# Four orders of the 21 products of a step in the experts' stage of a gated-attention and mixture-of-experts kernel

## The chip, the cores and the metric

The kernel runs on one core of a Trainium2 chip. The metric is the device time of one execution in microseconds (us), the median of several runs. Everything below is in fp32: each fp32 operand is split into a high and a low part of type fp32r, and a product of two split operands is three matmuls (high by high, and the two mixed terms).

## The reference

The part that the change touches is the last of three stages, the mixture of four experts. It takes 3072 tokens of 384 numbers from the stage before:

```python
def _moe2_ref(x, domain_probs, w1, w2) -> np.ndarray:
    N, D = x.shape
    E = w1.shape[0]
    p = domain_probs / (domain_probs.sum(-1, keepdims=True) + 1e-09)
    out = np.zeros((N, D), dtype=np.float32)
    for e in range(E):
        h = np.maximum(x @ w1[e], 0.0)
        out += p[:, e:e + 1] * (h @ w2[e])
    return out.astype(np.float32)
```

N is 3072, D is 384, E is 4, and the hidden width is 1024. Ahead of it stand a gated linear attention over 4 x 8 heads of 768 steps and a bilinear layer, `((x @ w1) * (x @ w2)) @ w3 @ w_out`.

## The kernel before

The attention and the bilinear layer run interleaved until some 417 us into the span. Then comes the experts' stage, in which TensorE (PE) alternates two kinds of matmul. This text calls them by the letters that the change uses:

- **U** (an "up" or first product, `up2_product`, the matmul at L1175): weights `we_hi` or `we_lo` (128x128), moving operand `x1_hi` or `x1_lo` (128x512), into bank 0 or 1. A step has 9 of them, three contraction tiles by three terms, in the order (x_hi, we_hi), (x_lo, we_hi), (x_hi, we_lo). U0, U1, U2 are the three terms.
- **D** (a "down" or second product, `down2_product`, the matmul at L1294): weights `h_hi` or `h_lo` (128x128, 128 tokens of the hidden activations), moving operand `we_hi` or `we_lo` (128x384). A step has 12 of them: four groups of 128 tokens (`sub` 0 to 3, each summing into its own bank out of 5, 2, 3, 4) by three terms. Sub 0 goes to bank 5, which the profile calls `score_banks`; the others are called `bank`.

For each expert `e` the tokens are taken in 12 tiles of 512 (`TILE2`), two tiles to a round of 16 steps (`STEPS2`), so a tile has 8 steps, one for each 128 hidden units. `step2(e, m, s, ahead)` issues the 12 D of step `s` and the 9 U of the step two further on (`ahead`), which write bank `s % 2`. PE executes its matmuls in the order in which they are written; this order is a literal loop in `step2`. Four experts with 48 tiles make 192 steps. The last two of expert 3 have nothing ahead and hold 12 D alone.

Around the step:

- When the last U of a step is done (`up_done`), ScalarE (ACT, L601) writes `h_hi` from the bank, then VectorE (DVE, L821) writes `h_lo`. PE waits for `h_lo_ready` at the start of the step that uses them, one full step after the U's end.
- In the last step of a tile (`s % 8 == 7`) each token group's last D increments `down_done`, and DVE adds the bank, scaled by the gate, into `total` (`add`, L1000), four adds in the order of the groups. In the first step of the next tile (`s % 8 == 0`) the first D of each group waits for `added`, its own group's add (L1291 ahead of it), since it overwrites the bank. These are the D of index 0, 3, 6 and 9.
- In the very first step, the first D of groups 1 to 3 also wait for `x1_lo_ready`, since their banks hold the end of the stage before, which DVE reads at L816.
- ScalarE and GpSimd (POOL) split the next expert's weights beside this; SyncE loads `x1` tiles two ahead and one weight set an expert.

Of the kernel before, what the change touches and what calls it, by code (L numbers as in the profile page):

```python
# [31 lines left out]
BATCH, HEADS, SEQ, D = 4, 8, 768, 48  # L32
# [11 lines left out]
KT, FT = DM // P, FF // P  # L44
# [11 lines left out]
SUBS = TILE2 // P  # L56
# [9 lines left out]
FOLD_BANKS = [0, 1, 2, 3, 4, 0, 1, 2]  # L66
SUM_BANKS = [5, 2, 3, 4]
TERMS = 3
assert KT * TERMS == SUBS * TERMS - TERMS
WARM = 6  # L70
CONSTANTS = 7
FLAG_STEP = STEPS1 - 4
# [16 lines left out]
def gated_attention_experts(nc, akq, v, akq_long, v_columns, w3T, w_out, wsets, probs, out):  # L89
# [4 lines left out]
    with ExitStack() as ctx:  # L94
# [924 lines left out]
        def _(pe):  # L1019
# [143 lines left out]
            def up2_waits(e, m, s):  # L1163
                u, f = divmod(s, FT)
                if f == 0:
                    pe.wait_ge(x1_loaded[u], 32 * (e * ROUNDS + m + 1))
                    if u == 0 and isinstance(m, int) and m == 0:
                        pe.wait_ge(piece_lo, PIECES * (e + 2))

            def up2_product(e, s, i):  # L1170

                u, f = divmod(s, FT)
                k, term = divmod(i, TERMS)
                cols = slice(k * FF + f * P, k * FF + (f + 1) * P)
                mm = pe.matmul(bank[s % 2][:, :], (we_hi if term < 2 else we_lo)[e % 2][:, cols], (x1_lo if term == 1 else x1_hi)[u][:, k, :],  # L1175
                               start=(i == 0), stop=(i == KT * TERMS - 1))
                if i == KT * TERMS - 1:
                    mm.then_inc(up_done, 1)
# [36 lines left out]
            for k in range(FT):  # L1215
# [5 lines left out]
                for f in range(FOLD_FIRST):  # L1221
# [5 lines left out]
                    else:  # L1227
                        i = k - SPLIT_FROM
# [55 lines left out]
            def down2_product(e, m, s, i):  # L1284

                u, f = divmod(s, FT)
                sub, term = divmod(i, TERMS)
                if term == 0 and e == 0 and s == 0 and sub >= 1:
                    pe.wait_ge(x1_lo_ready, X1_LOW_AHEAD + KT * (TILES1 * BATCH - 1) + sub)
                if term == 0 and f == 0:  # L1290
                    pe.wait_ge(added, SUBS * (e * TILES2 + 2 * m + u) + sub + 1)  # L1291
                rows = slice(sub * P, (sub + 1) * P)
                cols = slice(KT * FF + f * DM, KT * FF + (f + 1) * DM)
                mm = pe.matmul(bank[SUM_BANKS[sub]][:, 0:DM], (h_hi if term < 2 else h_lo)[:, s % 2, rows], (we_lo if term == 1 else we_hi)[e % 2][:, cols],  # L1294
                               start=(f == 0 and term == 0), stop=(f == FT - 1 and term == TERMS - 1))
                if f == FT - 1 and term == TERMS - 1:
                    mm.then_inc(down_done, 1)

            def step2(e, m, s, ahead):

                pe.wait_ge(h_lo_ready, STEPS2 * (e * ROUNDS + m) + s + 1)
                if ahead:
                    up2_waits(*ahead)
                ups = 0
                for i in range(SUBS * TERMS):
                    down2_product(e, m, s, i)
                    if ahead and i % SUBS >= 1:
                        up2_product(ahead[0], ahead[2], ups)
                        ups += 1

            def round2(e, m, following):

                for s in range(STEPS2):
                    if s + 2 < STEPS2:
                        step2(e, m, s, (e, m, s + 2))
                    else:
                        step2(e, m, s, following and (*following, s + 2 - STEPS2))
# [64 lines left out]
```

## Time and profile before

| | us |
|---|---|
| median of 3 runs | 1219.2 |
| lowest and highest | 1218.31 and 1219.39 |
| span of the profiled execution | 1217.6 |
| PE busy in it | 1212.3 |
| experts' stage in it, from the first D to the end | 419.6 to 1217.6 |
| one step of that stage | 4.16 |

The profiled execution has no measured time of its own beside its span. The median of the runs is 1.6 us above the span: what lies around the first and last instruction. In a timeline, the second column is how long a matmul was in the pipeline; matmuls overlap, so what a matmul costs is the distance from its start to the start of the next one.

### The profile page before, as it was taken

How to read it: one execution, taken by the hardware profiler on the slowest of the kernel's cores; microseconds unless marked ns; L12 is line 12 of the kernel's file. 1: busy time of each engine (PE TensorE's matmuls, PEld its weight loads, DVE VectorE, ACT ScalarE, POOL GpSimd, SP SyncE). 2: the span in 40 equal slices, each digit the busy share in tenths (PEclk: the TensorE clock that was granted, in tenths of full speed). 3: DMA queues.
4: the chain of work that ended last, by engine and by line, in shares of the span. 5: the costliest groups of instructions: out<-in, count | busy, mean ns of one | idle time of the engine just before them, and what ended most of it. 6: DMA issues, size and time to landing. Idle time of an engine off the chain costs nothing.

```text
span 1217.6 us, 18865 instructions
## 1 busy us (share of the span) xinstructions
PE 1212.3 (100%) x7740; PEld 1118.6 (92%) x7740; DVE 461.4 (38%) x886; ACT 281.7 (23%) x526; POOL 168.8 (14%) x148
## 2 busy tenths in 40 slices
PE   9999999999999999999999999999999999999998
PEld 8799999999999999999999999999999999999998
DVE  6997586586651122122222222222122222222222
ACT  3443333333333311111111111111111111111111
POOL 1132222222223520000000000000000000000000
PEclk9999999999999999999999999999999999999999
DMA  9644444544415331100141111123101111222201
GB/s 286 207 121 122 126 132 106 137 128 105 126 47 195 106 145 52 51 17 36 53 156 52 52 52 52 52 73 135 42 15 46 52 52 53 78 78 78 78 9 44
DMA packets 87543, 108.03 MB, mean 89 GB/s; under 512 B 38576, under 2 KB 57904, under 8 KB 86960
## 3 DMA queue, kind: packets, MB, share of 16 engines
q1 hardware_dynamic: 87184, 106.63, 28.0%
q8 instruction: 52, 0.85, 0.3%
q10 hardware_dynamic: 288, 0.39, 0.1%
q14 instruction: 19, 0.16, 0.0%
HBM read 86.29 MB, written 18.35 MB: 86 GB/s over the span
## 4 chain that ended last, share of the span: by engine, by line
PE 99%; DVE 0%; issue 0%; DVEq 0%; ACT 0%
PE bank L1175 33%; PE bank L1294 25%; PE bank L1022 9%; PE bank L1024 9%; PE bank L1023 9%; PE score_banks L1294 8%; PE bank L1063 2%; PE bank L1244 1%; PE score_banks L1084 1%; PE bank L1073 1%; PE score_banks L1047 1%; PE bank L1226 1%; PE bank L1214 0%; DVE total L1000 0%; PE bank L1031 0%
## 5 line engine op out<-in xcount | busy, mean ns | idle before, releaser
L821 DVE SCALAR_TENSOR_TENSOR h_lo<-bank,h_hi 128x512 fp32r<-128x512 f32 x192 | 132.8, 691 | 584.9 <-ACT h_hi L601 584.0
L601 ACT ACTIVATE h_hi<-bank 128x512 fp32r<-128x512 f32 x192 | 114.7, 597 | 661.7 <-PE bank L1175 661.7
L1175 PE MATMUL bank<-x_hi,we_lo 128*128 128x512 f32 x576 | 228.7, 397 | 0.0
L1175 PE MATMUL bank<-x_hi,we_hi 128*128 128x512 f32 x576 | 224.1, 389 | 0.0
L1175 PE MATMUL bank<-x_lo,we_hi 128*128 128x512 f32 x576 | 223.5, 388 | 0.0
L1294 PE MATMUL bank<-we_hi,h_hi 128*128 128x384 f32 x576 | 194.6, 338 | 0.0
L1294 PE MATMUL bank<-we_lo,h_hi 128*128 128x384 f32 x576 | 194.5, 338 | 0.0
L1294 PE MATMUL bank<-we_hi,h_lo 128*128 128x384 f32 x576 | 193.8, 336 | 0.0
L499 POOL TENSOR_TENSOR we_lo<-we_raw,we_hi (+1 forms) x48 | 60.9, 1289 | 527.8 <-ACT we_hi L562 527.8
L1175 PEld LDWEIGHTS bank<-x_hi,we_lo 128*128 128x128 f32 x576 | 108.3, 188 | 22.4
L1175 PEld LDWEIGHTS bank<-x_lo,we_hi 128*128 128x128 f32 x576 | 108.0, 188 | 22.7
L1022 PE MATMUL bank<-x,wb_hi 128*128 128x384 f32 x384 | 128.6, 335 | 0.0
L1024 PE MATMUL bank<-x,wb_lo 128*128 128x384 f32 x384 | 128.3, 334 | 0.0
L1023 PE MATMUL bank<-x,wb_hi 128*128 128x384 f32 x384 | 128.3, 334 | 0.0
L1294 PEld LDWEIGHTS bank<-we_hi,h_hi 128*128 128x128 f32 x576 | 108.3, 188 | 8.5
L1294 PEld LDWEIGHTS bank<-we_hi,h_lo 128*128 128x128 f32 x576 | 108.3, 188 | 8.4
L1175 PEld LDWEIGHTS bank<-x_hi,we_hi 128*128 128x128 f32 x576 | 108.3, 188 | 0.2
L1294 PEld LDWEIGHTS bank<-we_lo,h_hi 128*128 128x128 f32 x576 | 108.1, 188 | 0.0
L510 POOL TENSOR_TENSOR g_lo<-g_sb,g_hi 128x384 fp32r<-128x384 f32 x64 | 66.3, 1036 | 221.3 <-ACT g_hi L591 221.3
L811 DVE TENSOR_TENSOR g_sb<-a_sb,bank 128x384 f32<-128x384 f32 x64 | 35.3, 552 | 110.8 <-PE bank L1024 110.8
L1022 PEld LDWEIGHTS bank<-x,wb_hi 128*128 128x128 f32 x384 | 72.1, 188 | 0.2 <-issue 0.2
L1023 PEld LDWEIGHTS bank<-x,wb_hi 128*128 128x128 f32 x384 | 72.1, 188 | 0.1
(99 smaller groups left out, 1473.3 us busy)
## 6 DMA issues: line engine op xcount, KB each, us to landing
x_hi<-x_hi_spill SPq DMA_DIRECT2D x24, 768.0 KB, 4.8
x_lo<-x_lo_spill SPq DMA_DIRECT2D x24, 768.0 KB, 6.3
we_raw<-wset SPq DMA_DIRECT2D x4, 3072.0 KB, 10.0
inputs<-akq SPq DMA_DIRECT2D x24, 448.0 KB, 5.2
values<-v_rows SPq DMA_DIRECT2D x24, 256.0 KB, 3.7
inputs<-akq SPq DMA_DIRECT2D x24, 224.0 KB, 3.3
x_hi_spill<-x_hi_out SPq DMA_DIRECT2D x8, 576.0 KB, 4.3
x_lo_spill<-x_lo_out SPq DMA_DIRECT2D x8, 576.0 KB, 5.2
```

The lines of the kernel that those rows point to most:

```text
L499: pool.tensor_tensor(set_lo(n)[:, at], set_raw(n)[:, at], set_hi(n)[:, at], ALU.subtract).then_inc(piece_lo, 1)
L510: pool.tensor_tensor(g_lo[:, s % 2, :], g_sb[:, s % 2, :], g_hi[:, s % 2, :], ALU.subtract).then_inc(g_lo_ready, 1)
L601: act.activation(h_hi[:, s % 2, :], bank[s % 2][:, :], ACT.Relu).then_inc(h_hi_ready, 1)
L811: dve.tensor_tensor(g_sb[:, s % 2, :], a_sb[:, s % 2, :], bank[1][:, 0:TILE1], ALU.mult).then_inc(g_ready, 1)
L821: dve.scalar_tensor_tensor(out=h_lo[:, s % 2, :], in0=bank[s % 2][:, :], scalar=0.0, in1=h_hi[:, s % 2, :], op0=ALU.max, op1=ALU.subtract) ...
L1022: pe.matmul(dst, left[0], right[0], start=first, stop=False)
L1023: pe.matmul(dst, left[0], right[1], start=False, stop=False)
L1024: return pe.matmul(dst, left[1], right[0], start=False, stop=last)
L1047: mm = pe.matmul(bank[5 + half][rows, STATE_AT + i * D:STATE_AT + (i + 1) * D], keys_t[:, pair, rows], values[:, c % SLOTS, at], start=(i ...
L1063: mm = pe.matmul(bank[7][q * ODD:(q + 1) * ODD, (2 * row + g) * CHUNK:(2 * row + g + 1) * CHUNK], values[:, c % SLOTS, at], scores[:, row, ...
L1175: mm = pe.matmul(bank[s % 2][:, :], (we_hi if term < 2 else we_lo)[e % 2][:, cols], (x1_lo if term == 1 else x1_hi)[u][:, k, :], start=(i ...
L1294: mm = pe.matmul(bank[SUM_BANKS[sub]][:, 0:DM], (h_hi if term < 2 else h_lo)[:, s % 2, rows], (we_lo if term == 1 else we_hi)[e % 2][:, cols],
```

## The change

The loop over the 12 D of a step, in which a U followed each D whose index is 1, 2 or 3 modulo 4, becomes a loop over a string of letters, one string for each expert:

```diff
-assert KT * TERMS == SUBS * TERMS - TERMS
+ORDERS = [7 * "D" + "DU" + 4 * "DUU", 3 * "DDDUU" + "DDDUUU", 3 * "D" + 3 * "DDU" + 3 * "DUU", 3 * "D" + 3 * "DDDUUU"]
+assert all((weave.count("D"), weave.count("U")) == (SUBS * TERMS, KT * TERMS) for weave in ORDERS)
...
-                ups = 0
-                for i in range(SUBS * TERMS):
-                    down2_product(e, m, s, i)
-                    if ahead and i % SUBS >= 1:
+                ups = downs = 0
+                for product in ORDERS[e]:
+                    if product == "D":
+                        down2_product(e, m, s, downs)
+                        downs += 1
+                    elif ahead:
                         up2_product(ahead[0], ahead[2], ups)
                         ups += 1
```

Written out, the order of a step of 21 products is:

```
before, all experts  DDUDUDU DDUDUDU DDUDUDU
after, expert 0      DDDDDDDD U D UU D UU D UU D UU
after, expert 1      DDD UU DDD UU DDD UU DDD UUU
after, expert 2      DDDDD U DD U DD U D UU D UU D UU
after, expert 3      DDDDDD UUU DDD UUU DDD UUU
```

The kinds, counts, operands and order among the D and among the U are the same; every order ends with a U, as before. Other engines' instructions do not change.

```order
L1294 MATMUL score_banks<-we0_hi,h_hi 128x384
L1294 MATMUL score_banks<-we0_lo,h_hi 128x384
L1175 MATMUL bank0<-x1_0_hi,we0_hi 128x512
L1294 MATMUL score_banks<-we0_hi,h_lo 128x384
L1175 MATMUL bank0<-x1_0_lo,we0_hi 128x512
L1291 REGISTER_ALU
L1294 MATMUL bank2<-we0_hi,h_hi 128x384
L1175 MATMUL bank0<-x1_0_hi,we0_lo 128x512
L1294 MATMUL bank2<-we0_lo,h_hi 128x384
L1294 MATMUL bank2<-we0_hi,h_lo 128x384
```

The same place after; the lines have moved by one:

```order
L1295 MATMUL bank3<-we0_hi,h_hi 128x384
L1295 MATMUL bank3<-we0_lo,h_hi 128x384
L1176 MATMUL bank0<-x1_0_hi,we0_hi 128x512
L1295 MATMUL bank3<-we0_hi,h_lo 128x384
L1176 MATMUL bank0<-x1_0_lo,we0_hi 128x512
L1176 MATMUL bank0<-x1_0_hi,we0_lo 128x512
L1292 REGISTER_ALU
L1295 MATMUL bank4<-we0_hi,h_hi 128x384
L1176 MATMUL bank0<-x1_0_hi,we0_hi 128x512
L1176 MATMUL bank0<-x1_0_lo,we0_hi 128x512
```

Before these stand six D, of groups 0 and 1. So the first U stands behind eight D instead of two, and the first D of group 3 (the wait that is nearest to its release) is the 13th product of the step instead of the 16th.

On PE, the same step in the loop of expert 3, after:

```order
L1295 MATMUL bank2<-we1_hi,h_hi 128x384
L1295 MATMUL bank2<-we1_lo,h_hi 128x384
L1295 MATMUL bank2<-we1_hi,h_lo 128x384
L1176 MATMUL bank0<-x1_0_hi,we1_hi 128x512
L1176 MATMUL bank0<-x1_0_lo,we1_hi 128x512
L1176 MATMUL bank0<-x1_0_hi,we1_lo 128x512
L1292 REGISTER_ALU
L1295 MATMUL bank3<-we1_hi,h_hi 128x384
```

Before, this place reads as the first fence does, with `we1` for `we0`. Three terms of a token group now stand together, and three U of a contraction tile behind them.

## Rows read from the trace of the kernel before

**Rows 1.** The page: busy time by engine, granted PE clock, the chain that ended last.

```profile
PE 1212.3 (100%) x7740; PEld 1118.6 (92%) x7740; DVE 461.4 (38%) x886; ACT 281.7 (23%) x526; POOL 168.8 (14%) x148
PEclk9999999999999999999999999999999999999999
PE 99%; DVE 0%; issue 0%; DVEq 0%; ACT 0%
```

**Rows 2.** The waits: engine and line, who released it: us, times, longest.

```profile
ACT h_hi L601 <- PE bank L1175: 661.7, 192, 3.8
DVE h_lo L821 <- ACT h_hi L601: 584.0, 170, 3.7
...
PEld score_banks L1294 <- DVEq L1010: 0.4, 1, 0.4
```

**Rows 3.** The timeline of PE around one step: start us, us, engine, line, op.

```profile
548.69 0.34 PE L1294 MATMUL score_banks<-we_hi,h_hi 128*128 128x384 f32 x1
...
552.45 0.34 PE L1294 MATMUL bank<-we_hi,h_lo 128*128 128x384 f32 x1
552.62 0.40 PE L1175 MATMUL bank<-x_hi,we_lo 128*128 128x512 f32 x1
552.85 0.34 PE L1294 MATMUL score_banks<-we_hi,h_hi 128*128 128x384 f32 x1
553.03 0.34 PE L1294 MATMUL score_banks<-we_lo,h_hi 128*128 128x384 f32 x1
553.20 0.39 PE L1175 MATMUL bank<-x_hi,we_hi 128*128 128x512 f32 x1
553.43 0.34 PE L1294 MATMUL score_banks<-we_hi,h_lo 128*128 128x384 f32 x1
553.61 0.39 PE L1175 MATMUL bank<-x_lo,we_hi 128*128 128x512 f32 x1
553.84 0.34 PE L1294 MATMUL bank<-we_hi,h_hi 128*128 128x384 f32 x1
554.01 0.40 PE L1175 MATMUL bank<-x_hi,we_lo 128*128 128x512 f32 x1
554.24 0.34 PE L1294 MATMUL bank<-we_lo,h_hi 128*128 128x384 f32 x1
```

**Rows 4.** The same timeline, the first D of the second and of the 191st step.

```profile
423.89 0.34 PE L1294 MATMUL score_banks<-we_hi,h_hi 128*128 128x384 f32 x1
...
1210.13 0.34 PE L1294 MATMUL score_banks<-we_hi,h_hi 128*128 128x384 f32 x1
```

**Rows 5.** The same timeline where nine U, then nine 384-column products stand.

```profile
413.76 0.39 PE L1175 MATMUL bank<-x_hi,we_hi 128*128 128x512 f32 x1
413.98 0.39 PE L1175 MATMUL bank<-x_lo,we_hi 128*128 128x512 f32 x1
414.21 0.40 PE L1175 MATMUL bank<-x_hi,we_lo 128*128 128x512 f32 x1
414.45 0.40 PE L1175 MATMUL bank<-x_hi,we_hi 128*128 128x512 f32 x1
...
415.85 0.34 PE L1022 MATMUL bank<-g_hi,wp_hi 128*128 128x384 f32 x1
...
417.41 0.39 PE L1175 MATMUL bank<-x_hi,we_hi 128*128 128x512 f32 x1
```

**Rows 6.** The timeline with the weight loads (PEld), inside a step.

```profile
700.19 0.39 PE L1175 MATMUL bank<-x_hi,we_hi 128*128 128x512 f32 x1
700.19 0.19 PEld L1294 LDWEIGHTS bank<-we_hi,h_hi 128*128 128x128 f32 x1
700.41 0.34 PE L1294 MATMUL bank<-we_hi,h_hi 128*128 128x384 f32 x1
700.42 0.19 PEld L1175 LDWEIGHTS bank<-x_lo,we_hi 128*128 128x128 f32 x1
```

**Rows 7.** The timeline of the other engines around a tile's end: start us, us.

```profile
550.78 0.62 DVE L1000 SCALAR_TENSOR_TENSOR total<-bank,gate,total 128x384 f32 x1
551.99 0.62 DVE L1000 SCALAR_TENSOR_TENSOR total<-bank,gate,total 128x384 f32 x1 [0.59 <-PE bank L1294]
552.97 0.62 DVE L1000 SCALAR_TENSOR_TENSOR total<-bank,gate,total 128x384 f32 x1 [0.36 <-PE bank L1294]
553.05 0.60 ACT L601 ACTIVATE h_hi<-bank 128x512 fp32r<-128x512 f32 x1 [3.56 <-PE bank L1175]
553.68 0.69 DVE L821 SCALAR_TENSOR_TENSOR h_lo<-bank,h_hi 128x512 fp32r<-128x512 f32 x1
```

**Rows 8.** The timeline at the start of the stage: the last readers of banks 2 to 4.

```profile
418.19 1.49 DVE L816 TENSOR_TENSOR x_lo_out<-bank,x_hi_out 128x384 fp32r<-128x384 f32 x3 [0.82 <-ACT x_hi_out L597]
...
419.62 0.45 PE L1294 MATMUL score_banks<-we_hi,h_hi 128*128 128x384 f32 x1
```

## Prediction of the change's effect, made before its run

> **What bounds the kernel now.** I read the page first. PE is busy for 1212.3 of 1217.6 us, at full granted clock in every slice, and 99% of the chain that ended last is PE's [rows 1]. The waits say the same from the other side. The other engines wait for PE: ScalarE's h_hi waited 661.7 us in total for the first products, 192 times. The only wait of PE's weight loads in the experts' stage is 0.4 us, once, at its start [rows 2]. So a reordering on PE can matter in two ways only: PE may take longer or shorter for the same 21 products, or a wait may appear that is now satisfied in time.
>
> Next the timeline. A step of the experts' stage takes 4.16 us: one step's first D starts at 548.69, the next one's at 552.85 [rows 3]. This holds for the whole stage. The second step starts at 423.89 and the 191st at 1210.13 [rows 4], which is 786.24 us over 189 steps, 4.160 each, with loop ends, tile ends and changes of expert inside. There is no bubble anywhere to win back, so one nanosecond more or less a step, over the 190 changed steps, is 0.19 us.
>
> **What a product costs.** In the step, from start to start, a D costs 0.17 to 0.18 us and a U 0.22 to 0.23 [rows 3]. How do the two kinds cost when each stands alone in a run? The end of the stage before has that [rows 5]. Nine products of 384 columns run from 415.85 to 417.41, 1.56 us, 0.1733 each. They have D's shape and run just behind nine U, so I take them for D. Of the nine U the last six run from 414.45 to 415.85, 1.40 us, 0.2333 each. The first three run from 413.76 to 414.45, 0.69 us, 0.23 each: a U run starts a little cheap. Priced at the run's rates a step is 12 x 0.1733 + 9 x 0.2333 = 2.08 + 2.10 = 4.18 us. The mixed step takes 4.16, so mixing saves 20 ns of 4180. That is all that order has been worth so far.
>
> Why so little? Each weight load starts when the matmul ahead of it starts and no sooner: the load for the D at 700.41 starts at 700.19 together with the U, and the load for the next U at 700.42 with the D [rows 6]. A load takes 0.19 us and only one is ahead. Neither kind can then lend its slack to the other, and the sum is nearly independent of the order.
>
> The Trainium skill, page "TensorE: Matmul & The Clock Gate", section "Back-to-back issue gap", says that the spacing of a stream of load and matmul pairs is set by both, pipelined through a window of 64 entries. Taken at its word, loads could run several products ahead, a mix of U and D would even out, and runs of D would lose. The trace bears this out only for one load ahead, so by the rows the sum below stands, and by the page runs would cost up to what mixing now saves, which is the first rival.
>
> **The change, part by part.** Nothing is removed or added; 12 D and 9 U stand in another order in 190 steps, 48 for each of experts 0 to 2 and 46 for expert 3. The last two steps hold D alone and are the same as before.
>
> (a) *PE's own rate.* The known points of the saving against 4.18 are these. The step before has three groups of DDUDUDU and saves 20 ns, 6.7 for each [rows 3, 4]. The run of nine U and nine D takes 417.41 - 413.76 = 3.65 us against 9 x 0.4067 = 3.66, so it saves up to 10 ns (the rows' last digit is 10 ns) for one group of D followed by one group of U [rows 5]. Both fit this: about 6.7 ns are saved each time that U begins behind at least two D, and none where a lone D stands between two U. That is a fit to two patterns, not a mechanism, but it is the nearest thing that the rows offer. By it:
>
> - expert 0, one such place (eight D, then U): 4.180 - 0.007 = 4.173, +13 ns a step;
> - expert 1, four places (DDD each time): 4.180 - 0.027 = 4.153, -7 ns;
> - expert 2, three places (DDDDD, DD, DD): 4.160, 0;
> - expert 3, three places: 4.160, 0.
>
> The sum is 48 x (13 - 7) ns = +0.3 us. The four pairs behind a lone D in expert 0 and the three in expert 2 are patterns that the trace lacks. Their bounds: they save as much as any other start (6.7 ns each), or nothing. I take nothing, since the lone D of the step before, the nearest rows, fit that.
>
> (b) *The wait for the adds.* In a tile's first step the first D of each token group waits for that group's add. The tightest is group 3. Before, its last D starts at 552.45, its add starts at 552.97 and ends at 553.59, that is 0.74 us into the new step [rows 3, 7]. Its first D of the new tile is the 16th product. After, the group's last D stands ahead of two U in experts 0 and 2 and of three in 1 and 3, 0.6 or 0.9 us before the step's end instead of 0.4, so the add ends at about 0.5 or 0.3 us. The 10th D is wanted after 9 D and 3 U in experts 0 and 2, 9 x 0.173 + 3 x 0.23 = 2.25 us, and at some 2.9 us in the others. Spare time is over 1.7 us. The adds of groups 0 to 2 run inside the old tile's last step. The second starts at 550.78, 2.09 us into that step, and ends at 2.71 [rows 7]; the third can follow at once, since group 2's last D then stands at 2.3 us at the latest in the new orders, and ends at about 3.4 of the 4.16. So group 1 is released some 1.4 us and group 2 some 0.7 us before the new step, and the soonest that they are wanted is 0.52 and 1.04 us into it (expert 0, after three and after six D). The cost is nothing. Behind such a wait the whole rest of PE's queue would stand, and behind that ScalarE and VectorE.
>
> (c) *The wait for h_lo.* Every order ends with a U, as before. h_hi starts at 553.05, h_lo at 553.68 and ends at 554.37 [rows 7]; it is wanted at 552.85 + 4.16 = 557.01. The spare is 2.6 us and doesn't move.
>
> (d) *The very first step.* The first D's of groups 1 to 3 come earlier, but their banks' last readers end at 418.19 + 1.49 = 419.68, and the step's first D starts at 419.62 [rows 8]. Group 1's first D now comes 0.5 us after that. The cost is nothing.
>
> (e) The loads of x1, the weight splits and the adds follow semaphores that come at the end of a step or a tile, as before. Nothing moves that they wait for by more than 0.5 us, and none of them is on PE's path.
>
> **The sum.** 1217.6 + 0.3 = 1217.9 us of span, and with the 1.6 us around it 1219.5. I predict 1219.5, no difference that can be measured. A measurement of this kernel tells about 0.2%, 2.4 us, from no change; that would take 13 ns a step on average over all the changed steps.
>
> **Rivals.**
>
> 1. *Short alternation is what saves the 20 ns; groups pay the run's rates.* Each step then takes 4.18: + 0.020 x 190 = 3.8 us, 1223.0 and slower by 0.3%. For it speaks that the later U of a long run cost 0.233 and none in the mix costs that on average; three of the orders have pairs or triples. Against it, the first three U of the run together are still at 0.69 instead of 0.70 [rows 5], and no group here is longer than three. It decides for slower from an average step of 4.173 on, two thirds of the way. Chance 0.15.
>
> 2. *Every change from D to U saves 6.7 ns in the new patterns, behind a lone D too.* Expert 0 has five such places (4.147), expert 1 four (4.153), expert 2 six (4.140), expert 3 three (4.160): 48 x (-13 - 7 - 20) ns = -1.9 us, 1217.3. Against it: in the step before there are nine such changes and only 20 ns. This is still within 0.2%. Chance 0.15.
>
> 3. *Pairs of U are cheap in a way that neither run nor mix shows.* The first U of a run costs 0.22 [rows 5]; were all nine at 0.227 and all D at 0.1733, a step would be 4.12, -0.040 x 190 = -7.6 us, 1211.6. Against it, the third U of the run costs 0.24. Chance of getting a third of this or more, which is faster by over 0.2%: 0.06.
>
> 4. *A wait for an add takes over.* It needs the release of group 3 later than 2.25 us into a tile's first step; it costs what is beyond that, in 24 tiles. By (b) it is 1.7 us away. Chance 0.01.
>
> 5. *The order does nothing at all* and the step stays at 4.160 everywhere: 1219.2. Chance 0.15.
>
> **How the numbers follow.** The forecast has 0.48. With rivals 2 and 5 the chance of no measurable difference is 0.78, slower is rivals 1 and 4, 0.16, and faster is rival 3, 0.06. The range goes from rival 2, 1217.3, to rival 1, 1223.0; it leaves out rival 3, rival 4 and what noise lies beyond the ends.
>
> **What would show it.** In the profile after, PE's step by expert: the distance between first D's should be 4.17, 4.15, 4.16 and 4.16 us. If all are at 4.18, rival 1 holds. The wait view should still show one wait of PE for 0.4 us in the experts' stage and nothing behind the adds. A U's time in the group UUU should be 0.22, 0.23, 0.24 as at 413.76. The prediction is wrong if any order's step is off by over 20 ns from its figure, or if gaps stand ahead of the D that wait for adds.

## The result and the profile after

The changed kernel takes 1223.17 us, the median of 5 runs (1222.45 to 1223.43), against 1218.74 for the kernel before (1218.29 to 1219.39). The ratio is 1.0031, with a 95% interval of 1.002 to 1.0042. It is slower by 4.4 us. The profiled execution has a span of 1221.5 us, 3.9 more than before. The two figures differ because the profiled execution of the kernel before, with 1217.6 us, was some 0.5 us longer than the median of its runs gives (1218.74 less the 1.7 that lie around the span).

The page after, the lines that answer to [rows 1]:

```profile
PE 1216.2 (100%) x7740; PEld 1119.3 (92%) x7740; DVE 458.3 (38%) x886; ACT 282.0 (23%) x526; POOL 168.9 (14%) x148
PEclk9999999999999999999999999999999999999999
PE 99%; DVE 0%; issue 0%; DVEq 0%; ACT 0%
```

PE still sets the end, at full clock, and is busy for 3.9 us more than in [rows 1], with the same 7740 matmuls. The waits after, which answer to [rows 2]:

```profile
ACT h_hi L602 <- PE bank L1176: 665.2, 192, 3.8
...
PEld score_banks L1295 <- DVEq L1011: 0.4, 1, 0.4
```

The one wait of 0.4 us at the start of the experts' stage is still the only one there. So no wait was added, and the whole loss is in how long PE takes for the same products.

Where? The distances between the first D of successive steps tell it. These are rows of PE's timeline after (start us, us): the first D of the second step, of the first step of experts 1, 2 and 3, and of the 191st step. They answer to [rows 4].

```profile
424.02 0.34 PE L1295 MATMUL score_banks<-we_hi,h_hi 128*128 128x384 f32 x1
...
620.48 0.34 PE L1295 MATMUL score_banks<-we_hi,h_hi 128*128 128x384 f32 x1
...
820.15 0.34 PE L1295 MATMUL score_banks<-we_hi,h_hi 128*128 128x384 f32 x1
...
1020.81 0.34 PE L1295 MATMUL score_banks<-we_hi,h_hi 128*128 128x384 f32 x1
...
1213.99 0.34 PE L1295 MATMUL score_banks<-we_hi,h_hi 128*128 128x384 f32 x1
```

| expert | order | from to | steps | us a step | over before |
|---|---|---|---|---|---|
| 0 | 8D U D UU D UU D UU D UU | 424.02 to 620.48 | 47 | 4.180 | +20 ns |
| 1 | DDDUU three times, DDDUUU | 620.48 to 820.15 | 48 | 4.160 | 0 |
| 2 | 5D U DD U DD U D UU D UU D UU | 820.15 to 1020.81 | 48 | 4.180 | +20 ns |
| 3 | 6D UUU, DDD UUU twice | 1020.81 to 1213.99 | 46 | 4.200 | +40 ns |

Experts 0 to 3 lose 47 x 20, 0, 48 x 20 and 46 x 40 ns: 0.94 + 0.96 + 1.84 = 3.7 us. The second step's start is 0.13 us later than in [rows 4], which makes nearly all of the 3.9.

The order of expert 3 costs more than the rates of both runs together (4.18). A step of it, from the timeline:

```profile
1104.79 0.34 PE L1295 MATMUL score_banks<-we_hi,h_hi 128*128 128x384 f32 x1
1104.96 0.34 PE L1295 MATMUL score_banks<-we_lo,h_hi 128*128 128x384 f32 x1
1105.14 0.34 PE L1295 MATMUL score_banks<-we_hi,h_lo 128*128 128x384 f32 x1
1105.32 0.35 PE L1295 MATMUL bank<-we_hi,h_hi 128*128 128x384 f32 x1
1105.50 0.34 PE L1295 MATMUL bank<-we_lo,h_hi 128*128 128x384 f32 x1
1105.68 0.34 PE L1295 MATMUL bank<-we_hi,h_lo 128*128 128x384 f32 x1
1105.86 0.39 PE L1176 MATMUL bank<-x_hi,we_hi 128*128 128x512 f32 x1
...
1106.55 0.34 PE L1295 MATMUL bank<-we_hi,h_hi 128*128 128x384 f32 x1
...
1107.77 0.34 PE L1295 MATMUL bank<-we_hi,h_hi 128*128 128x384 f32 x1
...
1108.99 0.34 PE L1295 MATMUL score_banks<-we_hi,h_hi 128*128 128x384 f32 x1
```

The two groups DDDUUU last 1107.77 - 1106.55 = 1.22 us each, exactly the run rates (3 x 0.1733 + 3 x 0.2333). The six D from 1104.79 to 1105.86 take 1.07 us instead of 1.04. The fourth, fifth and sixth cost 0.18 us each, though nothing stands between them and they are D like the others.

The wait for the adds went as foreseen. These are the last add of a tile in expert 0, then two of PE's rows: the first D of the new tile's first step, and the D that waits. They answer to [rows 7].

```profile
520.05 0.62 DVE L1001 SCALAR_TENSOR_TENSOR total<-bank,gate,total 128x384 f32 x1 [0.97 <-PE bank L1295]
```

```profile
520.16 0.34 PE L1295 MATMUL score_banks<-we_hi,h_hi 128*128 128x384 f32 x1
...
522.42 0.34 PE L1295 MATMUL bank<-we_hi,h_hi 128*128 128x384 f32 x1
```

The last add ends at 520.67, 0.51 us into the step, and the 10th D starts at 522.42, 2.26 us into it.

### The profile page after: what moved, and what is told of

It reads as the page before. It is cut to its first block, busy times and chain, and to the rows that moved or that the text cites. A ratio compares the mean times of both kernels' runs of the same rounds, so it can differ in the third digit from the quotient of the medians.

```text
span 1221.5 us, 18865 instructions
## 1 busy us (share of the span) xinstructions
PE 1216.2 (100%) x7740; PEld 1119.3 (92%) x7740; DVE 458.3 (38%) x886; ACT 282.0 (23%) x526; POOL 168.9 (14%) x148
## 4 chain that ended last, share of the span: by engine, by line
PE 99%; DVE 0%; issue 0%; DVEq 0%; ACT 0%
PE bank L1176 33%; PE bank L1295 25%; PE bank L1023 9%; PE bank L1025 9%; PE bank L1024 9%; PE score_banks L1295 8%; PE bank L1064 2%; PE bank L1245 1%; PE score_banks L1085 1%; PE bank L1074 1%; PE score_banks L1048 1%; PE bank L1227 1%; PE bank L1215 0%; DVE total L1001 0%; PE bank L1032 0%
## 5 line engine op out<-in xcount | busy, mean ns | idle before, releaser
L1176 PE MATMUL bank<-x_lo,we_hi 128*128 128x512 f32 x576 | 226.4, 393 | 0.0
```

## The experiments

In each experiment but two, a kernel gives every expert an order of its own, so that one run prices four orders. A step's price is the distance between the first D of neighbouring steps inside an expert, averaged over the expert, since the rows shown have only 10 ns. It repeats to 1 ns from step to step, unless said otherwise. The exception is an expert's first step, which runs behind another order and can be up to 25 ns off. All runs had the full clock. The kernels of four orders were run once each; the two kernels of one order at the end, several times.

### Is it the order, or the expert?

The theory after the result was that the order alone sets the step. The rival was that the expert does (its weight buffer, or the loads and splits beside it).

```diff
-ORDERS = [7 * "D" + "DU" + 4 * "DUU", 3 * "DDDUU" + "DDDUUU", 3 * "D" + 3 * "DDU" + 3 * "DUU", 3 * "D" + 3 * "DDDUUU"]
+ORDERS = ["DDDDDDUUUDDDUUUDDDUUU", "DDDDDDDDUDUUDUUDUUDUU", "DDDUUDDDUUDDDUUDDDUUU", "DDDDDUDDUDDUDUUDUUDUU"]
```

> The four orders of the changed kernel given to other experts: expert 0 takes expert 3's, expert 1 takes 0's, expert 2 takes 1's, expert 3 takes 2's. Theory A, the order alone sets the step: 4.20, 4.18, 4.16, 4.18 us for experts 0 to 3, span about 1221.5. Theory B, the expert does (its weight buffer, or what the other engines do beside it): 4.18, 4.16, 4.18, 4.20 as in the changed kernel.

Measured: 4.200, 4.180, 4.160 and 4.180 us, span 1220.7. The steps add up as in the changed kernel (790.04 us from the second to the 191st, against 789.97); the span is 0.7 us shorter because the second step starts at 423.25 instead of 424.02. The price goes with the order. Two neighbouring steps of expert 0, which now has the order of expert 3:

```profile
507.25 0.34 PE L1295 MATMUL score_banks<-we_hi,h_hi 128*128 128x384 f32 x1
...
511.45 0.34 PE L1295 MATMUL score_banks<-we_hi,h_hi 128*128 128x384 f32 x1
```

This excludes the weight buffers and the work beside an expert.

### Is it the place in the step?

```diff
+ORDERS = ["DDDUUUDDDDDDUUUDDDUUU", "DDDUUUDDDUUUDDDDDDUUU", "DDDUUUDDDUUDDDUUDDDUU", "DDDDUUUDDDDUUUDDDDUUU"]
```

> Expert 0: DDDUUU DDDDDDUUU DDDUUU; expert 1: DDDUUU DDDUUU DDDDDDUUU (both are the changed kernel's expert 3 shifted against the step's start). Theory A, the cyclic order alone counts: 4.20 us both. Theory B, the place of the six D against the step's start (semaphore waits, h_hi and h_lo of the other engines) counts: 4.18 us or less, since the stall then has no cause. Expert 2: DDDUUU DDDUU DDDUU DDDUU, expert 1's order shifted: 4.16 by A. Expert 3: DDDDUUU three times: if the excess of 20 ns comes of the long D run behind UUU, between 4.18 and 4.24; if only of six D in a row, 4.18.

Measured: 4.200 and 4.200, 4.160, and in expert 3 steps of 4.213 and 4.187 us in turn, 4.200 on average. The shift changes neither price. The stall moves with the six D, to other banks, other operands, and another time against h_hi, h_lo and the adds. That excludes the semaphores and the other engines' work, and that one bank is slower than another. The change of bank still falls behind the third of the six D in both shifts; the next run moves that too.

Expert 3 is the most telling. Its input is one block, DDDDUUU, over and over, and the blocks come out unequal:

```profile
1114.85 0.34 PE L1295 MATMUL score_banks<-we_hi,h_hi 128*128 128x384 f32 x1
...
1115.55 0.39 PE L1176 MATMUL bank<-x_hi,we_hi 128*128 128x512 f32 x1
...
1116.24 0.34 PE L1295 MATMUL bank<-we_lo,h_hi 128*128 128x384 f32 x1
...
1116.95 0.40 PE L1176 MATMUL bank<-x_hi,we_hi 128*128 128x512 f32 x1
...
1117.65 0.34 PE L1295 MATMUL bank<-we_hi,h_lo 128*128 128x384 f32 x1
```

The first block lasts 1.39 us (four D in 0.70, three U in 0.69), the second 1.41 (0.71 and 0.70). They go on in turn, and since a step has three blocks, its length alternates too. At the run rates both would be 1.393. So the price of a block depends on what came before it. PE carries something over from block to block.

The changed kernel shows the same without any repetition, where the order changes. These are the first, second and third step of expert 3, the first behind the last step of expert 2:

```profile
1020.81 0.34 PE L1295 MATMUL score_banks<-we_hi,h_hi 128*128 128x384 f32 x1
...
1024.99 0.34 PE L1295 MATMUL score_banks<-we_hi,h_hi 128*128 128x384 f32 x1
...
1029.19 0.34 PE L1295 MATMUL score_banks<-we_hi,h_hi 128*128 128x384 f32 x1
```

The same 21 products in the same order take 4.18 us behind expert 2's order (4.177) and 4.20 behind their own. Expert 1's first step takes 4.155 (then 4.160) and expert 2's 4.197 (then 4.180); the same pairs of orders in the rotated kernel give 4.155 and 4.196. It isn't the change of expert itself: in the kernel below whose four experts all have expert 3's order, each expert's first step takes 4.200 like the rest.

### Do prices of blocks add?

The prediction had added up block prices. Five runs tried that.

```diff
+ORDERS = ["DDUDDUDDUDUDUDUDUDUDU", "DDDDUDUDUDUDUDUDUDUDU", "DUDUDUDUDDDDUDUDUDUDU", "DDUUDDUUDDUUDDUUDDDDU"]
```

> Four new patterns. Expert 0: DDU three times, then DU six times; expert 1: DDDD, then DU eight times, then U behind the last D; expert 2: DU four times, DDDD U, DU four times; expert 3: DDUU four times, DDDDU. By the prediction's fit (6.7 ns saved for each U group behind two or more D): 4.160, 4.173, 4.173, 4.147 us. By whole steps of 20 ns, as the changed kernel's rows show them: only 4.14, 4.16, 4.18 or 4.20 can come out.

Measured: 4.167, 4.200, 4.200 and 4.167 us. All four miss the fit's figures, by 7 to 27 ns. They miss the steps of 20 ns too: 4.167 is 6.7 ns above 4.160. Experts 1 and 2 have the same cyclic order and the same price. In them DU by itself costs 0.407, which is the sum of the run rates; plain alternation saves nothing. In both, the first three D of DDDD cost 0.174, 0.175 and 0.177 us and the fourth 0.185, though the bank changes ahead of the fourth D in expert 1 and ahead of the third in expert 2. So the change of bank isn't the cause either.

```diff
+ORDERS = ["DDDDDDDDDDDDUUUUUUUUU", "DDDDDDUUUUDDDDDDUUUUU", "DDDUDDDUUDDDUUUDDDUUU", "DDUUDDUUDDUUDDUDDDDUU"]
```

> Expert 0: twelve D, then nine U. Expert 1: DDDDDD UUUU DDDDDD UUUUU. Expert 2: DDD U DDD UU DDD UUU DDD UUU. Expert 3: DDUU DDUU DDUU DDU DDDDUU. If run rates alone price a run, expert 0 is 4.18 us (less 0.007); if a D run behind a U run of three or more pays 20 ns each time, expert 0 is 4.20, expert 1 is 4.22, expert 2 is 4.18, expert 3 is 4.16.

Measured: 4.173, 4.193, 4.173 and 4.193 us. The first is the figure of the run rates; the theory of 20 ns for each D run behind three or more U misses all four, by 7 to 33 ns. Twelve D and nine U cost what the run rates say less 7 ns, as the nine and nine in [rows 5] do. The stall is not a matter of long runs: none of the twelve D behind nine U is slow. In expert 1 the six D behind four U pay it, and the six behind five U don't.

Three further runs looked for shorter steps:

```diff
+ORDERS = ["DDUDUUDDDUUDDDUUDDDUU", "DDDUUDDUDDDUUDDUDDUUU", "DDUUDDDUUDDUDDDUUDDUU", "DDUUDDUUDDUUDDDUUDDDU"]
```

> Four further orders. The rows of the changed kernel and of the first experiments give block prices against run rates: DDDUU saves 7 ns, DDUDUDU saves 7, DDU saves up to 7, a closing UUU none. By those: DDUDUU DDDUU DDDUU DDDUU 4.153 us (if its first block saves as the others), DDDUU DDU DDDUU DDU DDUUU 4.153 to 4.160, DDUU DDDUU DDU DDDUU DDUU 4.153 to 4.160, DDUU DDUU DDUU DDDUU DDDU 4.160 to 4.167. If prices of blocks don't add, values from 4.15 to 4.20 come in no such order.

Measured: 4.153, 4.173, 4.160 and 4.167 us. Three are in their range; the second misses by 13 ns.

```diff
+ORDERS = ["DDUDUDUDDDUUDDDUUDDUU", "DDUDUDDUDUDDUDUDDUDUU", "DDUDDUDDDUUDDDUUDDUUU", "DDDDUUDDDUUDDUUDDUUDU"]
```

> Four more. DDUDUDU DDDUU DDDUU DDUU: 4.153 to 4.160 us by block prices. DDUDU three times, DDUDUDDUDUU in all twelve D and nine U: 4.153 to 4.167. DDUDDU DDDUU DDDUU DDUUU: 4.153 to 4.160. DDDDUU DDDUU DDUU DDUU DU: 4.160 to 4.173. If prices of blocks don't add: anything from 4.15 to 4.20.

Measured: 4.167, 4.153, 4.160 and 4.187 us. Two are in their range. The last is off by 13 ns and the first by 7.

```diff
+ORDERS = ["DDUDUUDDUDUDDDUUDDDUU", "DDUDUDDDUUDDUDUUDDDUU", "DDUDUDDUDUDDUDUUDDDUU", "DDDUUDDDUUDDDUUDDUUDU"]
```

> Four orders made of DDUDU, DDUDUU and DDDUU. If each of these blocks saves 7 ns against run rates, as the two orders of 4.153 us suggest, all four orders are at 4.147 to 4.153 us, the last (DDDUU three times, DDUU DU) at 4.153 to 4.160. If prices of blocks don't add, some are at 4.16 or above.

Measured: 4.160, 4.153, 4.153 and 4.160 us. The first two have the same four blocks in another sequence and differ by 7 ns. So prices of blocks don't add. That the misses are small here may come of the choice of blocks, which had been cheap together; this wasn't tried.

The 29 orders of these and the main kernels (a few are shifts of one another) lie between 4.153 and 4.200 us, 1.1% apart, and every one, once it repeats, is a multiple of 6.67 ns (4.153, 4.160, 4.167 and so on). So are the run rates of D and U, 26 and 35 times. The first step of an expert need not be (4.155, 4.197). The time of 16 columns at the granted 2.4 GHz is 6.67 ns; that the two belong together is a guess.

### What sets the price of a D?

The prediction had explained the small effect by the weight loads: one load ahead, 0.19 us long, about as long as a D. If a D lasts as long as its load, fewer columns in a D would save nothing. Experts 0 to 3 have the order of before and the changed kernel's of experts 0, 1 and 3.

```diff
+ORDERS = ["DDUDUDUDDUDUDUDDUDUDU", "DDDDDDDDUDUUDUUDUUDUU", "DDDUUDDDUUDDDUUDDDUUU", "DDDDDDUUUDDDUUUDDDUUU"]
...
+                width = DM if f == 0 else 320
+                cols = slice(cols.start, cols.start + width)
-                mm = pe.matmul(bank[SUM_BANKS[sub]][:, 0:DM], (h_hi if term < 2 else h_lo)[:, s % 2, rows], (we_lo if term == 1 else we_hi)[e % 2][:, cols],
+                mm = pe.matmul(bank[SUM_BANKS[sub]][:, 0:width], (h_hi if term < 2 else h_lo)[:, s % 2, rows], (we_lo if term == 1 else we_hi)[e % 2][:, cols],
```

> Experts 0 to 3 run the order of before, then the changed kernel's orders of experts 0, 1 and 3. Each D moves 320 columns instead of 384, except in a tile's first step; the last 64 output columns lack those products. Theory L, a D lasts as long as its weight load and its columns hide behind that: D stays at 0.173 to 0.175 us and the four steps at 4.16, 4.18, 4.16 and 4.20. Theory M, a D is paid by its columns: by the slope between 384 and 512 columns (0.1733 to 0.2333) it falls by 0.03 us, and a step by 12 x 0.03 = 0.36, to 3.80 to 3.84. If the differences of 20 ns between the orders come of D's and U's reads meeting, they change or vanish; if of the loads alone, they stay.

Measured, in steps with the narrow D: 3.820, 3.853, 3.820 and 3.847 us (the last 3.829 and 3.864 in turn). Behind a tile's first, wide step the next two differ in expert 0, 3.831 and 3.815, so what is carried over can outlast a whole step. The eight D of expert 1's order, the first, the second and the U behind the last of them:

```profile
684.32 0.31 PE L1297 MATMUL score_banks<-we_hi,h_hi 128*128 128x320 f32 x1
684.47 0.31 PE L1297 MATMUL score_banks<-we_lo,h_hi 128*128 128x320 f32 x1
...
685.49 0.40 PE L1176 MATMUL bank<-x_hi,we_hi 128*128 128x512 f32 x1
```

The weight loads of the second term of groups 1 to 3, in the same run (shortest, median and longest in ns):

```profile
L1297 PEld LDWEIGHTS bank<-we_lo,h_hi x576: 187/188/192, 422.0 to 1160.7; 128*128 128x128 f32 x192
```

Eight D in 1.17 us are 0.146 each, 0.027 less than at 384 columns, exactly what 64 columns take at 2.4 GHz. Theory L falls: the load does not hold a D back, although each load is still recorded with 0.188 us. The kernel before already spoke against it: there a D costs 0.173 and its load is recorded with 0.19. Theory M is right on the kind of bound, but it took the slope from D to U for the price of a column, 0.030 for 64; it is 0.027, and the rest of the distance from D to U is something that a U of 512 columns pays besides. So experts 1 and 3 lie above its 3.84. The differences between the four orders went from 0, 20, 0 and 40 ns to 0, 33, 0 and 27, so the loads alone, which are the same, don't make them.

### Does it hang on the length of a U?

```diff
-                mm = pe.matmul(bank[s % 2][:, :], (we_hi if term < 2 else we_lo)[e % 2][:, cols], (x1_lo if term == 1 else x1_hi)[u][:, k, :],
+                width = TILE2 if term == 0 else 448
+                mm = pe.matmul(bank[s % 2][:, 0:width], (we_hi if term < 2 else we_lo)[e % 2][:, cols], (x1_lo if term == 1 else x1_hi)[u][:, k, 0:width],
```

> The same four orders. The second and third term of each U moves 448 columns instead of 512; the last 64 tokens of each tile lack those terms. Both theories: such a U costs 0.20 instead of 0.23 us, since that is above a load, and the step falls by 6 x 0.027 to 6 x 0.030 = 0.16 to 0.18 us. Theory L leaves the differences between the four orders as they are (0, 20, 0, 40 ns); if they hang on U's length, they change.

Measured: 4.007, 3.993, 3.993 and 4.000 us, in the same four orders. The step falls by 0.153, 0.187, 0.167 and 0.200 us, where 0.16 to 0.18 was expected of every order. The ranking turns over: the order of before is now the slowest of the four, and the differences to it are 0, -13, -13 and -7 ns. No order is good or bad in itself, then. The ranking holds for the widths with which it was measured.

Another run made eight of the nine U as wide as a D; the matmul's line is changed as above:

```diff
+                width = TILE2 if i == 0 else DM
```

> The four orders of before and of the changed kernel's experts 0, 1 and 3, with eight of the nine U at 384 columns, as wide as a D; only a step's first U has 512. The last 128 tokens of each tile lack the products left out. If the differences between the orders come of U being longer than D, they shrink with it: 20 x 0.1733 + 0.227 to 0.233 us = 3.693 to 3.700 in all four orders, at most 7 ns apart. If they come of something that each product has whatever its width (its weight load, its bank, its place), they stay at 0, 20, 0 and 40 ns.

Measured: 3.713, 3.733, 3.720 and 3.713 us. Steps of experts 1 and 3:

```profile
675.91 0.33 PE L1296 MATMUL score_banks<-we_hi,h_hi 128*128 128x384 f32 x1
...
679.65 0.33 PE L1296 MATMUL score_banks<-we_hi,h_hi 128*128 128x384 f32 x1
```

```profile
1033.25 0.34 PE L1296 MATMUL score_banks<-we_hi,h_hi 128*128 128x384 f32 x1
...
1036.97 0.34 PE L1296 MATMUL score_banks<-we_hi,h_hi 128*128 128x384 f32 x1
```

Neither expectation holds. The spread shrinks from 40 to 20 ns but is not gone, and all four are 13 ns or more above the 3.700 that was expected at most. The order of expert 3, the worst at full width, is here the best together with that of before. That the one long U among twenty equal products does it isn't shown, since no run had all 21 equal. This run was inconclusive on the mechanism.

### The whole kernel on one order

```diff
+ORDERS = ["DDDDDDUUUDDDUUUDDDUUU", "DDDDDDUUUDDDUUUDDDUUU", "DDDDDDUUUDDDUUUDDDUUU", "DDDDDDUUUDDDUUUDDDUUU"]
```

> All four experts run DDDDDD UUU DDD UUU DDD UUU, the changed kernel's expert 3. If the order's price is the whole cause, and holds for every expert: a step of 4.200 us, 40 ns over before, 190 steps, + 7.6 us, a ratio of 1.0062. If the changed kernel's loss came of the changes between experts or of something else, it would stay near 1.003.

Measured: 1226.86 us against 1219.12, a ratio of 1.0062 with an interval of 1.0049 to 1.0076. The expected ratio was 1.0062. Its step is 4.200 in all four experts: from the second to the 191st step,

```profile
424.18 0.34 PE L1295 MATMUL score_banks<-we_hi,h_hi 128*128 128x384 f32 x1
...
1217.98 0.34 PE L1295 MATMUL score_banks<-we_hi,h_hi 128*128 128x384 f32 x1
```

793.80 us over 189 steps. The price of the order, 7.6 us over 190 steps, is the whole of the loss of 7.7, within the interval.

```diff
+ORDERS = ["DDUDUUDDDUUDDDUUDDDUU", "DDUDUUDDDUUDDDUUDDDUU", "DDUDUUDDDUUDDDUUDDDUU", "DDUDUUDDDUUDDDUUDDDUU"]
```

> All four experts run DDUDUU DDDUU DDDUU DDDUU, the shortest step found so far, 4.153 us. By the order's price: - 6.7 ns in 190 steps, - 1.3 us against before, a ratio of 0.9990, which the interval may not tell from no change. If it holds only in expert 0, where it was seen, the ratio is 0.9997 or more.

Measured: 1218.0 us against 1219.12, a ratio of 0.999 with an interval of 0.9981 to 0.9999.

```profile
423.89 0.34 PE L1295 MATMUL score_banks<-we_hi,h_hi 128*128 128x384 f32 x1
...
1208.87 0.34 PE L1295 MATMUL score_banks<-we_hi,h_hi 128*128 128x384 f32 x1
```

784.98 us over 189 steps are 4.153 each, 1.3 us under [rows 4] in all. It is the fastest kernel here, ahead of both, by about the smallest amount that these runs can tell.

## Why the prediction was right or wrong

**What bounds the kernel: right.** PE alone; a nanosecond a step was 0.19 us in the result, as the two kernels of one order show in both directions (+40 ns gave +7.7 us, -6.7 ns gave -1.1).

**The size and the sign.** 1219.5 was forecast and 1223.17 measured, 0.2 us beyond the range's upper end of 1223.0. The forecast was no measurable difference; it came out 0.3% slower, where 0.16 of the chance stood. Against the kernel before, +0.3 us was forecast and +4.4 measured. By its own sign, an order's step off by over 20 ns from its figure, the prediction is wrong: expert 3 is 40 ns off and expert 2 just 20. The range's upper end came from rival 1; what scatter lies beyond it was knowingly left out.

**(a) PE's own rate: this is the step that failed.** Its terms were +13, -7, 0 and 0 ns a step; measured are +20, 0, +20 and +40. The fit "6.7 ns saved each time U begins behind at least two D" matched both patterns that the trace held, and no new one of the four. It had one parameter and two points, one of which was rounded to 10 ns. What is wrong in it is more than the number. It priced blocks as if they added, and the alternating blocks of the run on places show that the same block has two prices. It also could give nothing above 4.18, since it knew only savings; expert 3 came out at 4.20. The text called it a fit and not a mechanism, but then let it choose the centre and gave it nearly half the chance.

**Why so little: right in size, wrong in cause.** The effect of order is small, 1.1% of a step from best to worst in 29 orders. The reason given for it, the weight load of 0.19 us with only one ahead, fell in the run with narrow D. A D is bound by its columns, 0.027 us for 64, and loads weren't in the way even at 0.146 us a product. In the Trainium skill, page "TensorE: Matmul & The Clock Gate", section "Back-to-back issue gap", load and matmul both set the spacing of their pairs. What the prediction drew from it, that a mix of U and D would even out and runs of D would lose, isn't what happened either: twelve D in a row make a step of 4.173 us, while one D and one U nearly throughout (the second and third order of the run on singles) make 4.200, as dear as any order here.

**(b) to (e), the waits: right.** The last add ends 0.51 us into the new tile's first step (foreseen 0.5) and the 10th D starts at 2.26 us (foreseen 2.25). The single wait of 0.4 us is unchanged.

**The rivals.** Rival 1 gave the total, 1223.0, to 0.2 us (its loss of 3.8 us against 4.4 measured, or 3.9 in the spans), and by its own test it is wrong: it said 4.18 in every step, and the steps are 4.18, 4.16, 4.18 and 4.20. Only their average is 4.18. This is worth noticing. The match was luck: by the total alone rival 1 would have been taken for shown. Rival 2 (a saving behind a lone D too) fell with the runs on singles, rival 3 (U at 0.227 throughout) too, rival 4 by the waits, rival 5 by the steps.

**What stays open.** The runs show that a step's price depends on the order, on the widths and on something that PE carries over from one block to the next. They exclude the expert's buffers, the banks, the place in the step, the semaphores, the other engines and a load that holds each D back. What is carried over, and whether the loads have a part in it, no run here shows.

## What to carry to other kernels

When PE is the bound and never waits, reordering independent matmuls can be worth little: here, with 384 and 512 columns, 1.1% of a step from worst to best. The profile of one order doesn't tell the price of another, and a fit of a few rows should not set the centre of a forecast. Such orders are quickly measured: give each repetition of a stage its own order and read the distance between its steps, which is exact to a nanosecond where whole runs differ by more. Compare the distances and not only the total, since opposite terms can add up to the figure of a wrong theory.

## What was not expected of the hardware

- A repeated block of seven matmuls (DDDDUUU) runs with two lengths in turn, 1.39 and 1.41 us, for a whole expert.
- In an unbroken row of four or six D the fourth can cost 0.185 us instead of 0.173, and the fifth and sixth 0.176 and 0.182. It depends on what ran before the row: rows of four behind one U and rows of six behind three or four U pay it, and in DDDDUUU every second row of four; rows of four, five and eight behind two U, of six behind five and of twelve behind nine don't.
- A D of 320 columns has 0.146 us from start to start, while its weight load is recorded with 0.188; as recorded, loads of neighbouring products overlap.
- The same 21 products in the same order take 4.177 us behind one order and 4.200 behind another. Once an order repeats, its step is a multiple of 6.67 ns, at full width in all 29 orders.
- The ranking of the orders changes with the number of columns.
